# Local and pooled attention by half batches, with the local softmax on ScalarE and VectorE

## Chip, cores and metric

The kernel runs on one core of a Trainium2 chip (trn2). The metric is the device time of one execution in microseconds, lower is better.

## The reference

The input has 4 batches, 8 heads, 576 tokens and 64 features a head. The first layer adds a pooled and a local attention, and two feed-forward layers follow:

```python
q_d = q.reshape(B, H, Sd, 4, D).mean(axis=3)      # k_d, v_d likewise
out_up = np.repeat(softmax(scale * q_d @ k_d.T) @ v_d, 4, axis=2)
mask = np.abs(pos[:, None] - pos[None, :]) < 4
scores = np.where(mask, scale * q @ k.T, -1e9)
a = np.exp(scores - max(scores)); a = a / (sum(a) + 1e-09)
x = out_up + a @ v                                # -> 2304 tokens x 512
h = x @ w_in; g = s * relu(h)**2 + b; x = g @ w_out          # 512 -> 2048 -> 512
out = (x @ w_a) * (x @ w_b) @ w2                             # 512 -> 1536 -> 512
```

## The kernel before

Five engines run programs of their own, in the written order, and meet at semaphores. The work has three parts.

**Attention** works on pairs of heads: `n` from 0 to 15, four pairs to a batch. A pair has three jobs: POOLED (all 144 groups), LOCAL0 and LOCAL1 (three windows of 96 queries each, a half of the tokens; a window sees 102 keys). `turn` transposes q and k on TensorE, `take_turn` evacuates on ScalarE, `sum_groups` pools on VectorE. A job then goes through `scores` (TensorE), `maxima` (VectorE: add the mask, find the maximum), for a local job `subtract` (GpSimd), `exps` (ScalarE), `weigh` (VectorE: sum, add 1e-9, reciprocal), `normalise` (GpSimd), `p_turn` (TensorE), `take_p` (ScalarE), `values` (TensorE) and `take_values` (VectorE, into `xf`).

**The first feed-forward layer** runs in 128 slots: 8 chunks `c` of 288 tokens by 16 blocks `f` of 128 hidden features. Every float32 product is made of three matmuls of a high and a low part, so weights (`split_w_hi`, `split_w_lo`) and activations are split first. A slot has `up_matmuls` (12 matmuls into the one bank HB), `take_relu` and `split_g_hi` on ScalarE, `square` and `split_g_lo` on VectorE, and `down_matmuls` of the slot two before it. `up_matmuls` of a slot waits for `take_relu` of the one before.

**The last layer** has 72 steps (`up_2`, `down_2`); its weight blocks are loaded and split in the last slots (0 to 5), behind them (6 to 8) and beside the first steps (9 to 11).

Before slot 0 a boot of 30 ticks makes all of batch 0: pairs 0 to 3 in two sets of buffers, six ticks apart, and splits six of the 16 weight blocks. In slots 0 to 95 pairs 4 to 15 are made in one set of buffers, eight slots (16 half slots `at`) to a pair. In each engine's loop `attention(n, at)` for the even half comes ahead of `up_matmuls`, `take_relu` and `square`; the one for the odd half comes behind these and ahead of `down_matmuls`, `split_g_hi` and `split_g_lo`. The pair's banks are used again and again, so a step also waits until the bank is free: `scores` of LOCAL1 in half slot 9 waits for `take_values` of POOLED in half slot 8 (the tensor `up`). SyncE issues nearly all DMAs, in written order too.

In the last slots store and load of the layer's result pass through DRAM (`o_dram`).

Of the kernel before, what the change touches and what calls it, by code (L numbers as in the profile page):

```python
# [4 lines left out]
P = 128  # L5
# [15 lines left out]
GW = NW // 2  # L21
SC = D ** -0.5


POOLED, LOCAL0, LOCAL1 = 0, 1, 2
JOBS = 3
NP = PAIRS * B

BOOT_SKEW = 6
BOOT_END = 11
BOOT_TICKS = BOOT_SKEW * (PAIRS - 1) + BOOT_END + 1
BOOT_BLOCKS = 6
BOOT_BLOCK_TICKS = (10, 14, 18, 22, 25, 28)

NCH = 2 * B
SLOTS = NCH * F1
GB = 3
# [8 lines left out]
STAGES = 3  # L48


def build(nc, q, k, v, w_in, w_out, s, b, w_a, w_b, w2, mask_in, identity, out, o_dram):
# [6 lines left out]
    with stack:  # L58
# [5 lines left out]


        boot = ExitStack()
        nat1 = sb(boot, "nat1", [WQ, 2, NW, 2 * D])
        vnat1 = sb(boot, "vnat1", [GH, 2, POOL * 2 * D])
        vwin1 = sb(boot, "vwin1", [WK, NW, 2 * D])
        vd1 = sb(boot, "vd1", [GH, 2, 2 * D])  # L70
        qT1 = sb(boot, "qT1", [P, S])
        kT1 = sb(boot, "kT1", [P, S + 2 * HALO])
        pooledT1 = sb(boot, "pooledT1", [P, 2, G])
        sm1 = sb(boot, "sm1", [WQ, 3, 2 * GW * WK])
        pts1 = sb(boot, "pts1", [WK, 2, GW * WQ])
        up1 = sb(boot, "up1", [P, G])
        sm0b = sb(boot, "sm0b", [WQ, 2 * GW * WK])
# [5 lines left out]
        nat0 = sb(first, "nat0", [WQ, 2, NW, 2 * D])  # L83
        vnat0 = sb(first, "vnat0", [GH, 2, POOL * 2 * D])
        vwin0 = sb(first, "vwin0", [WK, NW, 2 * D])
        vd0 = sb(first, "vd0", [GH, 2, 2 * D])
        qT0 = sb(first, "qT0", [P, S])
        kT0 = sb(first, "kT0", [P, S + 2 * HALO])
        pooledT0 = sb(first, "pooledT0", [P, 2, G])
        sm0 = sb(first, "sm0", [WQ, 2, 2 * GW * WK])  # L90
        pts0 = sb(first, "pts0", [WK, 2, GW * WQ])
        up0 = sb(first, "up0", [P, G])
        mask = sb(first, "mask", [WQ, NW, WK])
        ident = sb(first, "ident", [P, P])
        stat = sb(first, "stat", [WQ, 2, JOBS, 3, 2 * GW])
        xf = sb(first, "xf", [P, PAIRS, S])
# [40 lines left out]

        def block2(part, f):
# [25 lines left out]
        kT_clear = sem("kT_clear")  # L164
        vwin_clear = sem("vwin_clear")
        nat_in = [sem("nat_in0"), sem("nat_in1")]
        vnat_in = [sem("vnat_in0"), sem("vnat_in1")]
        vwin_in = [sem("vwin_in0"), sem("vwin_in1")]
# [4 lines left out]
        turn_ready = sem("turn_ready")  # L173
        turn_taken = sem("turn_taken")
        pooled = sem("pooled")
        s_ready = sem("s_ready")
        masked = sem("masked")
        mx_ready = sem("mx_ready")
        shift_ready = sem("shift_ready")
        sub_ready = sem("sub_ready")  # L180
        exp_ready = sem("exp_ready")
        sum_ready = sem("sum_ready")
        eps_ready = sem("eps_ready")
        rec_ready = sem("rec_ready")
        p_ready = sem("p_ready")
        pt_ready = sem("pt_ready")
        pt_taken = sem("pt_taken")
        v_half = sem("v_half")
        vd_ready = sem("vd_ready")
        o_ready = sem("o_ready")  # L190
        o_taken = sem("o_taken")
# [31 lines left out]
        def alone(n):  # L223
            return n < PAIRS

        def kit(n):
            return n % 2 if alone(n) else 0

        def before(n):

            return n - 2 if n <= PAIRS else n - 1

        def uses(n):

            return n // 2 + 1 if alone(n) else n - PAIRS + 3

        def job(n, kind):

            return JOBS * n + kind + 1 if n >= 0 else 0

        def local(n, kind):
            return 2 * n + kind if n >= 0 else 0

        def nat(n):
            return (nat0, nat1)[kit(n)]

        def vnat(n):
            return (vnat0, vnat1)[kit(n)]

        def vwin(n):  # L250
            return (vwin0, vwin1)[kit(n)]

        def vd(n):
            return (vd0, vd1)[kit(n)]

        def qT(n):
            return (qT0, qT1)[kit(n)]

        def kT(n):
            return (kT0, kT1)[kit(n)]  # L260

        def pooledT(n):
            return (pooledT0, pooledT1)[kit(n)]

        def pts(n):
            return (pts0, pts1)[kit(n)]

        def up(n):
            return (up0, up1)[kit(n)]

        def sm_flat(n, kind):
            if kit(n):
                return sm1[:, kind]
            if kind < LOCAL1:
                return sm0[:, kind]
            return sm0b[:, :] if alone(n) else sm0[:, 0]

        def sm_pooled(n):
            return sm_flat(n, POOLED)[0:GH, 0:4 * G].rearrange("p (e f c) -> p e f c", e=2, f=2)

        def sm_local(n, kind):
            return sm_flat(n, kind).rearrange("p (e u c) -> p e u c", e=2, u=GW)

        def rows_of(kind):
            return GH if kind == POOLED else WQ

        def blocks_of(kind):
            return 4 if kind == POOLED else 2 * GW

        def mx(n, kind):  # L290
            return stat[0:rows_of(kind), kit(n), kind, 0, 0:blocks_of(kind)]

        def shift(n):
            return stat[0:GH, kit(n), POOLED, 1, 0:4]

        def den(n, kind):
            return stat[0:rows_of(kind), kit(n), kind, 2, 0:blocks_of(kind)]


        def turn_bank(n, t):  # L300
            return 4 * kit(n) + t if alone(n) else (0, 1, 2, 0)[t]

        def s_bank(n, kind):
            return 4 * kit(n) + (2 if kind == LOCAL0 else 0) if alone(n) else 0

        def pt_bank(n):
            return 4 * kit(n) + 2 if alone(n) else 1

        def o_bank(n, kind):
            return 4 * kit(n) + (1 if kind == LOCAL0 else 0) if alone(n) else 0  # L310

        def boot_tick(at, tick_of):

            return [p for p in range(PAIRS) if at - BOOT_SKEW * p == tick_of]

# [3 lines left out]
        def _(sp):  # L319
            def load_qk(n):  # L320
                i, p = divmod(n, PAIRS)
                past(sp, turn_ready, 4 * before(n) + 4)
                for t, a in enumerate((q, k)):
                    for e in range(2):
                        src = a[i, 2 * p + e].rearrange("(w t) d -> t w d", t=WQ)
                        sp.dma_start(nat(n)[:, t, :, e * D:(e + 1) * D], src).then_inc(nat_in[kit(n)], 16)

            def load_v(n):
                i, p = divmod(n, PAIRS)
                past(sp, vd_ready, before(n) + 1)  # L330
                groups = v.rearrange("b h (f g r) d -> b f g h (r d)", f=2, r=POOL)
# [825 lines left out]
```

## Time and profile before

| | us |
|---|---|
| median of 3 runs | 1069.96 (1068.77 to 1071.46) |
| profiled execution | 1069.81 |
| its span, first to last instruction | 1068.0 |
| busy: TensorE matmul | 1009.2 (94%) |
| busy: VectorE | 442.6 (41%) |
| busy: ScalarE | 356.3 (33%) |
| busy: GpSimd | 159.4 (15%) |

The span is what the trace shows, the execution's own time lies 1.8 us above it. The boot ends near 79 us, the last slot near 596 us, and the last layer takes the rest. A busy share is a mean over these parts. A line of the trace's timeline gives the start, the duration and the instruction; the brackets behind it hold how long the engine had been idle and whose event ended that. TensorE's granted clock is 1.00 at 2.4 GHz and 0.50 at 1.2 GHz.

### The profile page before, as it was taken

What the parts mean: (1) busy time and instruction counts of PE and PEld (TensorE: products, weight loads), DVE (VectorE), ACT (ScalarE), POOL (GpSimd) and SP (SyncE); (2) the same over time, 40 slices, a digit from 0 to 9 for tenths busy, and PEclk for the clock granted to TensorE, in tenths of its full rate; (3) what the DMA queues carried; (4) which work ended last, traced back from release to release, by engine and by line L of the source; (5) the groups of instructions that cost most, each with busy time, mean ns of one, the idle gap of its engine ahead of it and who ended that gap; (6) DMA issues with size and microseconds to landing.
All of it is one profiled execution on the core that took longest, in us unless ns stands there. A gap on an engine that the chain in (4) does not pass through costs nothing.

```text
span 1068.0 us, 17004 instructions
## 1 busy us (share of the span) xinstructions
PE 1009.2 (94%) x6984; PEld 944.7 (88%) x6984; DVE 442.6 (41%) x800; ACT 356.3 (33%) x791; POOL 159.4 (15%) x126
## 2 busy tenths in 40 slices
PE   5678899999999999999999799999999999999997
PEld 4557889999999999999999699899899898998996
DVE  4768665565555655554345521211211212112111
ACT  3445444444344443344245421211211212212211
POOL 4545343122331223310000000000000000000000
PEclk9659999999999999999999899999999999999999
DMA  7343401121011210201033600010100100100000
GB/s 193 77 124 112 126 20 50 45 68 46 17 52 46 68 46 15 55 13 43 10 111 119 200 1 1 20 40 1 57 3 1 60 1 1 60 1 1 30 2 30
DMA packets 98829, 52.50 MB, mean 49 GB/s; under 512 B 60384, under 2 KB 92768, under 8 KB 98752
## 3 DMA queue, kind: packets, MB, share of 16 engines
q1 hardware_dynamic: 98608, 51.35, 17.3%
q8 instruction: 55, 0.90, 0.4%
q14 instruction: 22, 0.18, 0.1%
q10 hardware_dynamic: 144, 0.07, 0.0%
HBM read 41.97 MB, written 9.44 MB: 48 GB/s over the span
## 4 chain that ended last, share of the span: by engine, by line
PE 85%; DVE 6%; ACT 3%; POOL 3%; issue 2%; DMA 1%; SPq 0%; ACTq 0%; DVEq 0%; POOLq 0%
PE bank L667 28%; PE bank L632 18%; PE bank L617 17%; PE bank L681 13%; PE bank L546 2%; PE bank L493 2%; PE bank L517 2%; PE bank L467 1%; DVE relu L992 1%; POOL sm L1073 1%; PE bank L478 1%; POOL sm L1081 1%; PE bank L538 1%; POOL wx L1088 1%; PE bank L512 1%
## 5 line engine op out<-in xcount | busy, mean ns | idle before, releaser
L667 PE MATMUL bank<-x_hi,wx 128*128 128x384 f32 x1152 | 307.0, 337 | 11.8 <-DVE prod L1051 7.8
L632 PE MATMUL bank<-g_hi,wx 128*128 128x288 f32 x1024 | 234.2, 305 | 1.4 <-DVE o_sb L1004 1.4
L617 PE MATMUL bank<-wx 128*128 128x288 f32 x1536 | 230.7, 299 | 0.4 <-ACT relu L792 0.4
L667 PEld LDWEIGHTS bank<-x_hi,wx 128*128 128x128 f32 x1152 | 210.2, 188 | 17.3 <-issue 14.4
L617 PEld LDWEIGHTS bank<-wx 128*128 128x128 f32 x1536 | 211.8, 190 | 3.4 <-issue 2.8
L667 PE MATMUL bank<-x_lo,wx 128*128 128x384 f32 x576 | 193.5, 336 | 0.0
L632 PEld LDWEIGHTS bank<-g_hi,wx 128*128 128x128 f32 x1024 | 171.9, 189 | 9.5 <-issue 4.2
L1051 DVE TENSOR_TENSOR prod<-bank,a_sb 128x384 f32<-128x384 f32 x72 | 40.1, 558 | 314.5 <-ACT a_sb L854 314.5
L632 PE MATMUL bank<-g_lo,wx 128*128 128x288 f32 x512 | 151.5, 296 | 0.0
L992 DVE SCALAR_TENSOR_TENSOR relu<-relu,s_col 128x288 f32<-128x288 f32 x128 | 81.7, 638 | 166.4 <-ACT relu L792 166.2
L854 ACT ACTIVATE a_sb<-bank 128x384 f32<-128x384 f32 x72 | 35.3, 491 | 303.7 <-PE bank L667 303.7
L681 PE MATMUL bank<-wx,p_hi 128*128 128x512 f32 x432 | 134.4, 392 | 0.0
L667 PEld LDWEIGHTS bank<-x_lo,wx 128*128 128x128 f32 x576 | 108.6, 188 | 2.8
L792 ACT ACTIVATE relu<-bank 128x288 f32<-128x288 f32 x128 | 52.6, 411 | 173.7 <-PE bank L617 173.7
L632 PEld LDWEIGHTS bank<-g_lo,wx 128*128 128x128 f32 x512 | 96.7, 189 | 0.0
L797 ACT ACTIVATE g_hi<-relu,b_col 128x288 fp32r<-128x288 f32 x128 | 68.5, 535 | 80.4 <-DVE relu L992 80.4
L1081 POOL TENSOR_TENSOR sm<-sm,stat 96x612 f32<-96x612 f32 (+1 forms) x46 | 56.3, 1224 | 246.5 <-DVE stat L900 246.5
L681 PEld LDWEIGHTS bank<-wx,p_hi 128*128 128x128 f32 x432 | 80.1, 188 | 13.4
L996 DVE SCALAR_TENSOR_TENSOR g_lo<-relu,b_col,g_hi 128x288 fp32r<-128x288 f32 x128 | 70.6, 552 | 41.7 <-ACT g_hi L797 41.7
L681 PE MATMUL bank<-wx,p_lo 128*128 128x512 f32 x216 | 85.5, 396 | 0.0
L1054 DVE TENSOR_TENSOR p_lo<-prod,p_hi 128x384 fp32r<-128x384 f32 x72 | 40.2, 559 | 42.6 <-ACT p_hi L857 42.6
L857 ACT ACTIVATE p_hi<-prod 128x384 fp32r<-128x384 f32 x72 | 37.8, 526 | 46.2 <-DVE prod L1051 46.2
(67 smaller groups left out, 821.4 us busy)
## 6 DMA issues: line engine op xcount, KB each, us to landing
nat<-in_q SPq DMA_DIRECT2D x32, 144.0 KB, 2.9
nat<-in_k SPq DMA_DIRECT2D x32, 144.0 KB, 3.2
vnat<-in_v SPq DMA_DIRECT2D x32, 144.0 KB
o_transposed<-o_sb SPq DMA_DIRECT2D x8, 576.0 KB, 3.2
o_raw<-o_transposed SPq DMA_DIRECT2D x6, 768.0 KB, 4.7
out<-y SPq DMA_DIRECT2D x18, 256.0 KB, 2.2
vwin<-in_v SPq DMA_DIRECT2D x32, 120.0 KB
raw<-in_moe_w_a SPq DMA_DIRECT2D x12, 256.0 KB, 3.1
```

The source lines that it names most:

```text
L617: mm = nc.tensor.matmul(HB[:, 0:HALF], wi(w, kd, f), xs(x, c % 2)[:, kd], start=(kd == 0 and j == 0), stop=(kd == KD - 1 and j == 2))
L632: mm = nc.tensor.matmul(ACC[o][:, 0:HALF], wo(w, f, o), g[:, slot % GB, :], start=(f == 0 and j == 0), stop=(f == F1 - 1 and j == 2))
L667: mm = nc.tensor.matmul(dst[:, 0:CH2], wab(w, f, j * KD + kd), x[:, kd, :], start=(kd == 0 and m == 0), stop=(kd == KD - 1 and m == 2))
L681: mm = nc.tensor.matmul(ACC[tt], x[:, f % GB, tt * P:(tt + 1) * P], rows2(w, f), start=(f == 0 and m == 0), stop=(f == F2 - 1 and m == 2))
L792: nc.scalar.activation(relu[:, slot % 2, :], HB[:, 0:HALF], ACT.Relu).then_inc(r_ready, 1)
L797: nc.scalar.activation(g_hi[:, slot % GB, :], relu[:, slot % 2, :], ACT.Identity, bias=b_col[:, 0:1])\
L857: nc.scalar.activation(p_hi[:, f % GB, :], prod[:, f % 2, :], ACT.Copy).then_inc(ph_ready, 1)
L992: nc.vector.scalar_tensor_tensor(r, r, s_col[:, 0:1], r, ALU.mult, ALU.mult).then_inc(q_ready, 1)
L996: nc.vector.scalar_tensor_tensor(g_lo[:, slot % GB, :], relu[:, slot % 2, :], b_col[:, 0:1], g_hi[:, slot % GB, :].bitcast(f32), ALU.add, ...
L1051: nc.vector.tensor_tensor(prod[:, f % 2, :], bank[:, 1, 0:CH2], a_sb[:, f % 2, :], ALU.mult)\
L1054: nc.vector.tensor_tensor(p_lo[:, f % GB, :], prod[:, f % 2, :], p_hi[:, f % GB, :].bitcast(f32), ALU.subtract).then_inc(pl_ready, 1)
L1081: nc.gpsimd.tensor_tensor(x, x, d, ALU.mult).then_inc(p_ready, 1)
```

## The change

The work of attention is cut anew. A unit `u` is a pair of heads over half a batch (288 tokens): its three local windows and its 72 pooled queries. There are 32; units 4c to 4c+3 feed chunk `c`. The first units of a pair (`leads`) also transpose all its keys and sum its pooled values, which are kept for the second half. The boot makes units 0 to 3 only, in four buffer sets (34 ticks), with four weight blocks; units 4 to 31 are made in the slots, eight half slots to a unit, each over some 15 ticks, so two units are in work at a time. Weight blocks 4 to 15 are split one to a slot in slots 0 to 11.

Scores are kept negated. The local maximum becomes a minimum and enters `exp` as a bias, so ScalarE makes six exponentials of 96x102 instead of one of 96x612 and `subtract` on GpSimd goes. The 1e-9 stands in a 103rd column that the sum takes in. The local `normalise` moves from GpSimd to VectorE, next to the reciprocal. `up` is taken by ScalarE (`take_up`) in place of VectorE. Loads of the windows are joined, the first loads are shared between two queues, and blocks 6 to 11 of the last layer are split behind the steps.

The core of the diff:

```diff
+NU = PAIRS * NCH
+SETS = PAIRS
+PER_UNIT = 2 * F1 // PAIRS
+LEAD = 3
 BOOT_SKEW = 6
+BOOT_TICKS = 34
+BOOT_BLOCK_TICKS = (-14, -9, -5, -3)
+EARLY2 = 6
...
+        def bank_before(u):
+            return max(u - 1, 0) if u <= PAIRS else u
+        def at_tick(g, boot_tick, tick):
+            first = [u for u in range(PAIRS) if BOOT_SKEW * u - BOOT_TICKS + boot_tick == g]
+            return first + [u for u in range(PAIRS, NU) if PER_UNIT * (u - PAIRS) - LEAD + tick == g]
...
         @block.tensor
+            def scores(u):
+                _, h, p = place(u)
+                at = base(u)
+                pe.wait_ge(kp_ready, pair(u) + 1)
+                pe.wait_ge(qp_ready, u + 1)
+                past(pe, ptl_taken, bank_before(u))
+                past(pe, o_taken, bank_before(u))
...
+            def attention(g):
+                for u in at_tick(g, 12, 7):
+                    values(u)
+                for u in at_tick(g, 0, -5):
+                    if leads(u):
+                        turn_k(u)
+                for u in at_tick(g, 1, -4):
+                    turn_q(u)
+                for u in at_tick(g, 3, 0):
+                    scores(u)
+                for u in at_tick(g, 11, 6):
+                    turn_pooled(u)
+                for u in at_tick(g, 10, 6):
+                    turn_local(u)
...
             for slot in range(SLOTS):
-                c, f = divmod(slot, F1)
-                n, at = PAIRS + slot // 8, 2 * (slot % 8)
-                attention(n, at)
-                if slot > 0:
-                    up_matmuls(c, f)
-                attention(n, at + 1)
+                attention(2 * slot)
+                up_matmuls(*divmod(slot, F1))
+                attention(2 * slot + 1)
                 if slot >= 2:
                     down_matmuls(*divmod(slot - 2, F1))
...
         @block.scalar
+            def exp_local(u):
+                act.wait_ge(mnl_ready, u + 1)
+                for j in range(2 * GW):
+                    x = kits[kit(u)]["sml"][:, j, 0:WK]
+                    done = nc.scalar.activation(x, x, ACT.Exp, bias=mnl(u)[:, j:j + 1], scale=-1.0)
+                done.then_inc(el_ready, 1)
...
+            def take_up(u):
+                act.wait_ge(o_ready, u + 1)
+                past(act, o_taken, before(u))
+                nc.scalar.activation(kits[kit(u)]["up"][:], bank[:, base(u) + 2, HALF:HALF + GH], ACT.Copy,
+                                     scale=1.0 / POOL).then_inc(up_taken, 1)
...
+            def attention(g):
+                for u in at_tick(g, 13, 8):
+                    take_up(u)
+                for u in at_tick(g, 14, 9):
+                    split_x_hi(u)
+                for u in at_tick(g, 12, 6):
+                    take_pooled(u)
+                for u in at_tick(g, 11, 6):
+                    take_local(u)
+                for u in at_tick(g, 1, -5):
+                    if leads(u):
+                        take_k(u)
+                for u in at_tick(g, 2, -4):
+                    take_q(u)
+                for u in at_tick(g, 6, 2):
+                    exp_local(u)
+                for u in at_tick(g, 8, 3):
+                    exp_pooled(u)
...
-            for f in range(6, 9):
-                split_w2_hi(f)
             take_acc(NCH - 1)
...
         @block.vector
+            def weigh_local(u):
+                dve.wait_ge(el_ready, u + 1)
+                nc.vector.tensor_reduce(denl(u), kits[kit(u)]["sml"][:], X, ALU.add).then_inc(sum_ready, 1)
+                dve.wait_ge(sum_ready, u + 1)
+                nc.vector.reciprocal(denl(u), denl(u)).then_inc(recl_ready, 1)
+                dve.wait_ge(recl_ready, u + 1)
+                x = kits[kit(u)]["sml"][:, :, 0:WK]
+                d = denl(u).unsqueeze(2).to_broadcast([WQ, 2 * GW, WK])
+                nc.vector.tensor_tensor(x, x, d, ALU.mult).then_inc(pl_done, 1)
+
+            def take_values(u):
+                dve.wait_ge(up_taken, u + 1)
+                past(dve, x_hi, u - 1)
+                past(dve, x_lo, u - 1)
+                dst = xf[:, u % 2, :].rearrange("p (g r) -> p g r", r=POOL)
+                src = bank[:, base(u) + 2, 0:HALF].rearrange("p (g r) -> p g r", r=POOL)
+                add = kits[kit(u)]["up"][:].unsqueeze(2).to_broadcast([P, GH, POOL])
+                nc.vector.tensor_tensor(dst, src, add, ALU.add).then_inc(o_taken, 1)
...
+            def attention(g):
+                for u in at_tick(g, 14, 8):
+                    take_values(u)
+                for u in at_tick(g, 15, 9):
+                    split_x_lo(u)
+                for u in at_tick(g, 1, -4):
+                    if leads(u):
+                        sum_k(u)
+                for u in at_tick(g, 2, -3):
+                    sum_q(u)
+                for u in at_tick(g, 4, 0):
+                    minima(u)
+                for u in at_tick(g, 8, 3):
+                    weigh_local(u)
+                for u in at_tick(g, 9, 4):
+                    weigh_pooled(u)
...
         @block.gpsimd
-            def subtract(n, kind):
...
-            def normalise(n, kind):
...
+            def attention(g):
+                for u in at_tick(g, 10, 5):
+                    normalise_pooled(u)
+                for u in at_tick(g, 5, -2):
+                    if leads(u):
+                        sum_v(u)
```

On SyncE `load_q`, `load_k`, `load_v` and `load_vwin` of unit u+1 are issued by the same ticks: queries, keys and values at tick -3 of unit u, windows at tick 8 of unit u. `store_o` of the last chunk is now issued ahead of the loads of blocks 9 to 11, not of 11 alone.

## Rows read from the trace of the kernel before

**Rows 1.** The page, part 1: busy us (share of the span) xinstructions.
```profile
PE 1009.2 (94%) x6984; PEld 944.7 (88%) x6984; DVE 442.6 (41%) x800; ACT 356.3 (33%) x791; POOL 159.4 (15%) x126
```

**Rows 2.** Timeline of TensorE, steady slots: start us, us, instruction.
```profile
255.93 0.91 PE L467 MATMUL bank<-ident,nat 96*128 96x96 f32 x9
289.24 0.91 PE L467 MATMUL bank<-ident,nat 96*128 96x96 f32 x9
...
492.89 1.75 PE L617 MATMUL bank<-wx 128*128 128x288 f32 x12
496.08 1.75 PE L617 MATMUL bank<-wx 128*128 128x288 f32 x12
```

**Rows 3.** Waits of TensorE, 78 to 200 us: total, times, longest.
```profile
PE bank L478 <- DVE pooledT L868: 3.3, 2, 1.9
PE bank L493 <- DVE up L907: 3.0, 2, 1.7
...
PE bank L617 <- ACT relu L792: 0.4, 1, 0.4
```

**Rows 4.** Timeline, boot: first transposes, first and last minimum search of a half.
```profile
6.82 2.15 PE L467 MATMUL bank<-ident,nat 96*128 96x96 f32 x12 [6.82 <-DMA nat<-in_k]
...
13.38 0.79 DVE L890 TENSOR_REDUCE stat<-sm 96x6 f32<-96x612 f32 x1
...
66.54 0.79 DVE L890 TENSOR_REDUCE stat<-sm 96x6 f32<-96x612 f32 x1
```

**Rows 5.** Forms by line, 200 to 600 us: xcount, busy us, mean ns.
```profile
L890 DVE TENSOR_REDUCE stat<-sm 96x6 f32<-96x612 f32 x18 | 14.2, 786 | 0.6
L888 DVE TENSOR_TENSOR sm<-bank,mask 96x612 f32<-96x612 f32 x18 | 14.0, 780 | 0.0
L719 ACT ACTIVATE sm<-sm 96x612 f32<-96x612 f32 x18 | 12.7, 704 | 0.0
L713 ACT ACTIVATE sm<-bank,stat 72x144 f32<-72x144 f32 x32 | 11.6, 370 | 3.4 <-DVE stat L877 3.4
L776 ACT ACTIVATE wx<-xf 128x288 fp32r<-128x288 f32 x24 | 10.4, 433 | 0.0
L868 DVE TENSOR_REDUCE pooledT<-kT 128x144 f32<-128x576 f32 x8 | 6.0, 748 | 0.0
```

**Rows 6.** Timeline of TensorE, first slots; in brackets the idle before.
```profile
85.11 1.85 PE L617 MATMUL bank<-wx 128*128 128x288 f32 x12
...
99.08 0.77 PE L493 MATMUL bank<-kT,qT 64*96 64x102 f32 x12 [1.75 <-DVE up L907]
```

**Rows 7.** Timeline around 254 us, TensorE, then ScalarE, then VectorE.
```profile
253.57 0.72 PE L546 MATMUL bank<-pts,vwin 102*64 102x96 f32 x12
...
253.68 0.41 ACT L792 ACTIVATE relu<-bank 128x288 f32<-128x288 f32 x1 [0.59 <-PE bank L617]
...
254.13 0.52 DVE L992 SCALAR_TENSOR_TENSOR relu<-relu,s_col 128x288 f32<-128x288 f32 x1 [1.02 <-ACT relu L792]
254.56 0.45 DVE L917 TENSOR_TENSOR xf<-bank,up 128x288 f32<-128x288 f32 x1
```

**Rows 8.** Timeline of VectorE: a 96x6 operation while GpSimd splits a block.
```profile
96.49 2.13 DVE L898 TENSOR_SCALAR stat<-stat 96x6 f32<-96x6 f32 x1
```

**Rows 9.** Windows of TensorE: length, busy (x), granted clock, DMA share, GB/s.
```profile
121.00:124.00 3.00, 1.09 (x11) 1.00 0.20 77
...
126.00:128.00 2.00, 2.00 (x10) 0.50 1.10 255
```

**Rows 10.** Timeline of TensorE, start of the last stage.
```profile
606.97 0.66 PE L667 MATMUL bank<-x_hi,wx 128*128 128x384 f32 x1 [6.56 <-DVE prod L1051]
...
613.95 0.41 PE L667 MATMUL bank<-x_hi,wx 128*128 128x384 f32 x1 [1.26 <-DVE prod L1051]
```

**Rows 11.** The chain that ended last, same place: start us, us, what.
```profile
606.97 5.73 PE bank L667 x24
...
620.43 4.18 PE bank L667 x24
```

More of the change, by code:

```diff
@@ L306, in pt_bank, with place, leads, pair @@
[L306 to L314, printed above, removed]
+        def place(u):
+            return u // (2 * PAIRS), u // PAIRS % 2, u % PAIRS
+        def leads(u):
+            return place(u)[1] == 0
+        def pair(u):
+            i, _, p = place(u)
+            return PAIRS * i + p
@@ L319, in _, with load_q @@
         def _(sp):
[L320 to L330, printed above, removed]
+            def load_q(u, heads=range(2)):
+                i, h, p = place(u)
+                past(sp, q_turned, before(u))
+                for e in heads:
+                    src = q[i, 2 * p + e, h * HALF:(h + 1) * HALF].rearrange("(w t) d -> t w d", t=WQ)
+                    sp.dma_start(kits[kit(u)]["natq"][:, :, e * D:(e + 1) * D], src).then_inc(q_in[kit(u)], 16)
@@ L457, in _ @@
         def _(pe):
-            def turn(n, t):
-                if t == 0:
-                    pe.wait_ge(nat_in[kit(n)], 64 * uses(n))
-                    past(pe, o_taken, job(before(n), LOCAL1))
-                    past(pe, pt_taken, job(before(n), LOCAL1))
-                if t == 3 and not alone(n):
-                    pe.wait_ge(turn_taken, 4 * n + 1)
-                for u in range(GW):
-                    mm = nc.tensor.transpose(bank[:, turn_bank(n, t), u * WQ:(u + 1) * WQ],
-                                             nat(n)[:, t // 2, GW * (t % 2) + u, :], ident[0:WQ, 0:WQ])
-                mm.then_inc(turn_ready, 1)
@@ new lines, in turn_local @@
+            def turn_local(u):
+                pe.wait_ge(pl_done, u + 1)
+                if not alone(u) and u + 1 < NU:
+                    pe.wait_ge(q_taken, u + 2)
+                for e in range(2):
+                    for w in range(GW):
+                        mm = nc.tensor.transpose(bank[0:WK, base(u) + e, w * WQ:(w + 1) * WQ],
+                                                 kits[kit(u)]["sml"][:, GW * e + w, 0:WK], ident[0:WQ, 0:WQ])
+                mm.then_inc(ptl_ready, 1)
@@ new lines, in take_q, with exp_pooled @@
+            def take_q(u):
+                act.wait_ge(q_turned, u + 1)
+                past(act, sl_ready, before(u))
+                nc.scalar.activation(kits[kit(u)]["qT"][:], bank[:, turn_q_bank(u), 0:HALF], ACT.Copy, scale=-SC)\
+                  .then_inc(q_taken, 1)
+            def exp_pooled(u):
+                act.wait_ge(shift_ready, u + 1)
+                past(act, ptp_ready, before(u))
+                for e in range(2):
+                    done = nc.scalar.activation(kits[kit(u)]["smp"][:, e], bank[0:GH, base(u) + 2, e * G:(e + 1) * G],
+                                                ACT.Exp, bias=shift(u)[:, e:e + 1], scale=-1.0 / POOL ** 2,
+                                                accum_out=denp(u)[:, e:e + 1])
+                done.then_inc(ep_ready, 1)
@@ L1036, in _ @@
                         split_w2_lo(f // 2 - 2)
-            for f in range(6, 9):
-                split_w2_lo(f)
             take_acc(NCH - 1)
@@ L1124 @@
+            for g in range(-BOOT_TICKS, 0):
+                attention(g)
+                if g in BOOT_BLOCK_TICKS and BOOT_BLOCK_TICKS.index(g) % 2 == 1:
+                    split_w_lo(BOOT_BLOCK_TICKS.index(g))
+            for slot in range(SLOTS):
+                c, f = divmod(slot, F1)
+                attention(2 * slot)
+                attention(2 * slot + 1)
+                if c == 0 and f + BOOT_BLOCKS < F1 and f % 2 == 1:
+                    split_w_lo(f + BOOT_BLOCKS)
 _INS = ['q', 'k', 'v', 'moe_w_in', 'moe_w_out', 'moe_s', 'moe_b', 'moe2_w_a', 'moe2_w_b', 'moe2_w_out']
```

886 lines of the change are left out of this document (328 added, 558 removed).

## The prediction

> **What bounds the kernel now.** I read the engine shares first, then the waits of TensorE, then whole slots. TensorE is busy for 94% of the span [rows 1], so in the main loops the time is TensorE's own work plus the gaps in it. A slot without attention takes 496.08 - 492.89 = 3.19 us. Eight slots with one pair's attention take 289.24 - 255.93 = 33.31 us [rows 2], so a pair costs 33.31 - 8 x 3.19 = 7.79 us of TensorE, and there is no gap in that stretch. The pair is spread over 11 interludes between products; its matmuls alone add up to about 6.2 us in the same stretch, which leaves about 0.14 us for each change between attention and products (an estimate from these rows).
>
> The other losses lie in three places. First, the boot, where VectorE, ScalarE and GpSimd pass small tiles to each other: the first search for a local maximum ends at 14.2 us, the last but none of the eight starts at 66.54 [rows 4], and the third up product, the first from which the loop is full, starts at 85.11 [rows 6]. Second, the first twenty slots: seven kinds of waits, 11.8 us between 78 and 200 us [rows 3], of which 10.0 lie behind 85.11, and about 1.7 us for matmuls at half clock behind the longest gap [rows 9]. Third, the entry of the last stage: a gap of 6.56 us and then matmuls that begin at 0.66 us apiece instead of 0.41 [rows 10].
>
> **The boot shrinks: -24 us.** The change does only the first half of batch 0 before slot 0: four units in four buffer sets, each half a pair. Per unit VectorE has the mask (0.78), the minimum (0.79), a reduction of the keys (0.75) [rows 5], a sum of the minimum's size, and smaller ones: I take 6.3 us with the new multiply, which bounds a unit from below. The chain is longer than that, because the engines work in written order. From one unit's local minimum to the next one's: six exponentials 1.5, take_up 0.2, take_k 0.6, sum_k 0.7, take_values 0.4, x_hi 0.4, take_q 0.3, sum_q 0.4, weigh_local 1.9, x_lo 0.4, weigh_pooled 0.4, mask and minimum 1.6, and thirteen handovers of some 0.07: 9.7 us. The first minimum ends earlier than now, since only the first keys must be there before the first transpose (now all four loads are, at 6.8 us [rows 4]): I take 11.1. Three units on, with 2 us for the weight splits in between, is 42. From the last unit's minimum to the third up product come its exponentials, weights, transposes, values, take_values and split (14 us, unit 4's scores and minima are queued ahead of take_values on VectorE), then two up products that no down product covers (5 us): 61 us, against 85.11 now, so -24.1. A chain of 7.5 us a unit gives 53, one of 12 gives 68: the term lies in -32 to -17.
>
> **More attention in the loop: +13.5 us.** Now 12 pairs run in the slots; after, 28 half units (14 pairs). The matmuls of a unit are half a pair's, except that the pooled values take four products of 72 columns instead of two of 144 (0.05 us more); interludes fall from 11 to 9 for two units. Two units: 6.33 + 9 x 0.14 = 7.6, a unit 3.8 (3.6 to 4.1). Behind the third up product: 28 x 3.8 less 1.4 for unit 4's queries and scores in the boot = 105; now 12 x 7.79 less 2.0 = 91.5. Bounds +8 to +22.
>
> **The exchanges of engines: nothing on the path.** The two GpSimd operations on each half's local block (subtract, normalise) go. The subtraction becomes the bias of six exponentials over 102 columns in place of one over 612 (0.704 us [rows 5]). No row has 96x102; the pooled ones of 72x144 take 0.37 us, and 288 against 612 elements (0.43, 0.70) give 0.8 ns an element [rows 5], so I take 0.3 us each, with starts 0.25 apart: 1.5 us in all. Bounds 1.2 and 2.2 (six times 0.37). The multiply on VectorE is a 96x612 operation like the mask: 0.79. ScalarE then works about 9 and VectorE about 11 us in a unit's 16.6 us, so neither is the bound. From the scores (tick 0) to the transposes (tick 6) lie three slots, about 12 us, for mask to multiply of some 7 us plus their places in the queues; placing them against relu, square and g_hi, I find the pooled probabilities ready 1.7 us before TensorE asks. If the exponentials took 2.2 this cover falls to 1.0 and still holds. The local epsilon in a 103rd column saves a small operation off the path.
>
> The page "ScalarE: Activation LUTs" of the Trainium skill (Rules for kernel authors) budgets about 0.3 us per ACTIVATE plus 0.83 ns per element. By that six would cost 2.3 us, which speaks against this part; the boot would be some 3 us longer and the sum 1093.
>
> **The handover between units: +40 us.** This term decides. Unit u+1's scores sit at tick 0, an odd half slot, behind the up product of that slot, and wait for o_taken of unit u, because their banks are the same. o_taken comes from take_values at tick 8, the same half slot. values of unit u are done before that up product, but take_up is queued on ScalarE behind take_relu of the slot, and take_values on VectorE behind square, and both of these wait for the up product. So TensorE finishes it and then waits for relu, square, take_values. The same three stand in a row now: TensorE starts its next group at 253.57, relu starts 253.68, square 254.13, take_values 254.56 and ends 255.01 [rows 7]. Now nobody waits for them. With 0.05 us to TensorE that is 255.06 - 253.57 = 1.49 us; take_up (0.2 us, from 253.98) hides beside square. Units 5 to 31 pay it: 27 x 1.49 = 40.2 us. The row nearest to it is the wait of LOCAL1's scores for up in the first slots, 1.75 us [rows 6], where VectorE was also held back by GpSimd. Queued behind the waiting scores is the down product of the slot, which has been ready for long, so it can't fill the gap. Bounds 1.35 and 2.0 us: +36 to +54.
>
> **The first slots: -2.7 us.** The weight splits keep their place (one in each of slots 0 to 11, now ten in slots 2 to 11). A 96x6 operation of VectorE took 2.13 us while GpSimd was splitting [rows 8]. GpSimd's other work is mostly gone, but each unit's chain is longer, and normalise_pooled stands behind a split. I take 9 us for 11.7 (4 to 16: -8 to +4).
>
> **The last stage: -6.9 us.** Blocks 6 to 8 are no longer split ahead of the first a_sb; they follow step by step beside 6 us of products. The 6.56 us gap becomes 1.26, as at the next step [rows 10], and the half clock goes with it (5.73 against 4.18 us for 24 matmuls [rows 11]): 5.3 + 1.55. Loads move on SP too: store_o now waits ahead of three block loads rather than one, and these are due many steps later. Bounds -7 to -5.
>
> **Sum.** -24.1 + 13.5 + 40.2 - 2.7 - 6.9 = +20.0 us. The profiled execution took 1069.8 us (span 1068.0, 1.8 around it), the median of three is 1069.96. Forecast 1069.8 + 20 = 1090 us.
>
> **Rivals.** (1) *No gap at the handover.* take_values is done before TensorE asks, or the gap only moves one that would be there anyway: 1090 - 40 = 1050, faster. For it: in 200 to 300 us every such dependence of the present order is met in time. Against it: now the evacuation sits in an even half slot, ahead of square in VectorE's queue; in the change it is behind it, in program order, which engines don't pass by. 12%.
> (2) *The gaps drop the clock.* Behind a gap of 1.91 us the granted clock stood at 0.50 in 126 to 128 us, that is 1.2 GHz [rows 9]; 1.7 us were lost. At each of 27 handovers that is +46: 1136. Against it: four other gaps of 1.3 to 1.8 us, the one in rows 6 among them, were followed by matmuls at 2.4 GHz. Decides if a 1.5 us gap is enough. 4%.
> The page "TensorE: Matmul & The Clock Gate" (the HAM clock gate) holds that the half rate is the idle default and activity lifts it; gaps this short beside dense work would then seldom do it.
> (3) *A shorter boot than thought.* If VectorE's own work bounds it (6.3 us a unit) the loop is full at 50, the sum 1079: inside the main case.
>
> **Chances.** The main case 82%, its own range 1067 to 1115 from the bounds above, which don't all fall on one side. Rival 1: 12%, rival 2: 4%, another way 2%. The range 1068 to 1115 leaves out both rivals and little of the main case. This kernel's runs tell a change from none at about 0.3%, 3.2 us: faster 0.14, same 0.04, slower 0.82.
>
> **What would show it.** The waits of TensorE list the scores line waiting for xf from take_values, 27 times, about 1.5 us, evenly until some 540 us. Four slots with one unit take 18 us, not 16.6. The third up product starts near 61. The entry to the last stage has no gap over 1.5 us. POOL's busy time falls to well under half. I am wrong in the main point if the scores start right behind the up product.

## The result, and the profile after

The changed kernel takes 1088.68 us (median of four runs, 1086.81 to 1088.80) against 1070.71 us before on the same chip (four runs, 1068.77 to 1073.02). The ratio is 1.0163, interval 1.0143 to 1.0184: slower by 1.6%. The profiled execution took 1088.69 us, its span 1086.9. The forecast was 1090.

The page of the changed kernel, parts 1 and 5 (busy us, share, instructions; then a group with its busy time, mean ns, and the idle time before it with what ended it):

```profile
PE 1001.5 (92%) x7112; PEld 941.4 (87%) x7112; DVE 447.1 (41%) x866; ACT 387.5 (36%) x983; POOL 76.4 (7%) x80
...
L498 PE MATMUL bank<-pooledk,pooledq 64*72 64x144 f32 x128 | 30.0, 318 | 48.1 <-DVE xf L862 42.7
```

Against [rows 1], GpSimd's busy time has halved (159.4 to 76.4), ScalarE works 31 us more, and TensorE is busy for 7.7 us less in a span 18.9 us longer: the time is in gaps. Where the gaps are is in the waits of TensorE in the changed kernel (total, times, longest):

```profile
PE bank L498 <- DVE xf L862: 42.7, 27, 2.1
PE bank L484 <- ACT kT L658: 5.8, 5, 2.9
PE bank L523 <- POOL smp L983: 5.5, 5, 1.5
...
PE bank L533 <- DVE sml L853: 3.7, 1, 3.7
...
PE bank L627 <- DVE prod L958: 2.5, 2, 1.3
```

L498 is the first matmul of a unit's scores, L862 is take_values. It waits 27 times, once for each of units 5 to 31. The timeline of the changed kernel at one of these handovers (start, us, instruction, idle before):

```profile
310.31 1.86 PE L585 MATMUL bank<-wx 128*128 128x288 f32 x12
312.21 0.41 ACT L744 ACTIVATE relu<-bank 128x288 f32<-128x288 f32 x1 [3.21 <-PE bank L585]
312.52 0.22 ACT L697 ACTIVATE up<-bank 128x72 f32<-128x72 f32 x1
312.66 0.52 DVE L907 SCALAR_TENSOR_TENSOR relu<-relu,s_col 128x288 f32<-128x288 f32 x1 [3.10 <-ACT relu L744]
313.09 0.45 DVE L862 TENSOR_TENSOR xf<-bank,up 128x288 f32<-128x288 f32 x1
313.69 0.31 PE L498 MATMUL bank<-pooledk,pooledq 64*72 64x144 f32 x1 [1.51 <-DVE xf L862]
```

The up product ends, relu starts, square starts, take_values starts behind it, and only then may the scores begin. It is the row of [rows 7] with somebody waiting at its end. Both engines in between are otherwise idle (3.21 and 3.10 us before their instructions).

The boot and the entry of the last stage answer to [rows 4], [rows 6], [rows 10] and [rows 11]. The timeline of the changed kernel, first and last minimum search of the boot, and the third up product:

```profile
11.28 0.79 DVE L831 TENSOR_REDUCE stat<-sml 96x6 f32<-96x612 f32 x1
...
40.84 0.79 DVE L831 TENSOR_REDUCE stat<-sml 96x6 f32<-96x612 f32 x1
...
66.44 1.86 PE L585 MATMUL bank<-wx 128*128 128x288 f32 x12
```

The chain that ended last in the changed kernel, at the entry of the last stage (start, us, what):

```profile
616.90 5.00 PE bank L597 x36
621.90 4.21 PE bank L627 x24
627.36 4.42 PE bank L627 x24
```

The third up product starts at 66.44 instead of 85.11 [rows 6], and the last stage has no gap like the 6.56 us of [rows 10]: the 24 matmuls of its second step, which stood behind that gap, take 4.42 us, where [rows 11] had 5.73.

### The profile page after: what moved, and what is told of

Same layout as the page of the kernel before. It is cut to its first block, busy times and chain, and to the rows that moved or that the text cites. A ratio compares the mean times of both kernels' runs of the same rounds, so it can differ in the third digit from the quotient of the medians.

```text
span 1086.9 us, 17677 instructions
## 1 busy us (share of the span) xinstructions
PE 1001.5 (92%) x7112; PEld 941.4 (87%) x7112; DVE 447.1 (41%) x866; ACT 387.5 (36%) x983; POOL 76.4 (7%) x80
## 4 chain that ended last, share of the span: by engine, by line
PE 88%; DVE 5%; ACT 4%; issue 2%; POOL 1%; DMA 1%; DVEq 0%; ACTq 0%; POOLq 0%
PE bank L627 28%; PE bank L597 19%; PE bank L585 18%; PE bank L641 13%; PE bank L550 2%; PE bank L498 2%; PE bank L533 2%; PE bank L504 1%; DVE xf L862 1%; PE bank L543 1%; ACT relu L744 1%; PE bank L523 1%; DVE sml L853 1%; PE bank L471 1%; ACT sml L679 1%
## 5 line engine op out<-in xcount | busy, mean ns | idle before, releaser
L907 DVE SCALAR_TENSOR_TENSOR relu<-relu,s_col 128x288 f32<-128x288 f32 x128 | 73.1, 571 | 123.9 <-ACT relu L744 123.9
L498 PE MATMUL bank<-pooledk,pooledq 64*72 64x144 f32 x128 | 30.0, 318 | 48.1 <-DVE xf L862 42.7
L498 PEld LDWEIGHTS bank<-pooledk,pooledq 64*72 64x72 f32 x128 | 15.3, 153 | 55.0 <-issue 55.0
L961 DVE TENSOR_TENSOR p_lo<-prod,p_hi 128x384 fp32r<-128x384 f32 x72 | 40.2, 558 | 42.5 <-ACT p_hi L801 42.5
```

Of the source, the lines that this page charges most:

```text
L498: return nc.tensor.matmul(bank[0:GH, at + 2, e * G:(e + 1) * G], kits[kit(u)]["pooledq"][rows, :], pooledk[rows, p, :], start=True, stop=True)
L907: nc.vector.scalar_tensor_tensor(r, r, s_col[:, 0:1], r, ALU.mult, ALU.mult).then_inc(q_ready, 1)
L961: nc.vector.tensor_tensor(p_lo[:, f % GB, :], prod[:, f % 2, :], p_hi[:, f % GB, :].bitcast(f32), ALU.subtract).then_inc(pl_ready, 1)
```

## The experiments

In each, `...` stands for lines that stay. A ratio is against the kernel before on the same chip; for differences among the variants I use their medians. They ran on different chips, on which the kernel before had medians of 1068.4 to 1070.7 us, so a difference under some 2 us can't be told.

**1. Both evacuations half a slot earlier (take_early).** The theory: take_values stands behind square in VectorE's queue, so it comes late for a bank that TensorE asks for at once. If both steps move one tick ahead, nothing stands behind them and the gap goes.

```diff
-                for u in at_tick(g, 13, 8):
+                for u in at_tick(g, 13, 7):
                     take_up(u)
...
-                for u in at_tick(g, 14, 8):
+                for u in at_tick(g, 14, 7):
                     take_values(u)
```

> The changed kernel with one edit: take_up and take_values of a unit at tick 7 instead of 8, that is in the even half slot, ahead of take_relu and square in their engines' queues. Theory (handover): o_taken comes while the up product still runs, the 27 waits of the scores for take_values (42.7 us in the profile of the changed kernel) go, nothing takes their place: 1089 - 43 = 1046 us, below the kernel before. Rival (the gaps only hide others, TensorE is then late at the next wait, for the pooled probabilities or for relu): the waits reappear under another name and the time falls by under 15 us, to 1074 or more.

Measured 1041.02 us, ratio 0.9735 (0.9720 to 0.9749): 47.7 us below the changed kernel and 2.7% below the kernel before. The timeline of this run at a handover:

```profile
301.73 1.86 PE L585 MATMUL bank<-wx 128*128 128x288 f32 x12
301.85 0.23 ACT L697 ACTIVATE up<-bank 128x72 f32<-128x72 f32 x1 [1.44 <-PE bank L550]
302.11 0.46 DVE L862 TENSOR_TENSOR xf<-bank,up 128x288 f32<-128x288 f32 x1 [1.15 <-ACT up L697]
303.52 0.34 PE L498 MATMUL bank<-pooledk,pooledq 64*72 64x144 f32 x1
```

take_values now runs beside the up product and is done 0.95 us before the scores start. The wait of L498 for L862 isn't in the list of this run, and between 200 and 560 us the only wait of TensorE left is one of 0.3 us. So nothing was queued behind the gap to take its place. The gaps were 42.7 us, and half clock behind two of them in the first slots (below) is about 3 us more. The other 2 us are in the handovers too. From the scores at 151.59 to those at 546.23 us the changed kernel takes 394.6 us, with 22 handovers; this run takes 359.8 for the same stretch (138.96 to 498.80). That is 1.58 us for each, 0.07 more than the gap in the trace, because here the scores begin 0.07 us before the up product ends.

**2. Which of the two must move.** take_up alone, then take_values alone.

```diff
-                for u in at_tick(g, 13, 8):
+                for u in at_tick(g, 13, 7):
                     take_up(u)
```

> The changed kernel with take_up alone moved to tick 7 (ahead of take_relu on ScalarE), take_values left at tick 8 behind square. Theory: relu, square and take_values are what TensorE waits for, take_up only lay beside square; the 27 gaps stay at 1.5 us: 1089 us, within 2. Rival (take_up is part of the chain): it falls by 27 x 0.2 = 6 us.

Measured 1087.86 us, ratio 1.0174 (1.0156 to 1.0193); the wait is 42.9 us, as in the changed kernel. The copy on ScalarE was hidden beside square, as the prediction said.

```diff
-                for u in at_tick(g, 14, 8):
+                for u in at_tick(g, 14, 7):
                     take_values(u)
```

> The changed kernel with take_values alone at tick 7 (ahead of square on VectorE), take_up left behind take_relu on ScalarE. Theory: the chain becomes relu, take_up, take_values, by the starts in the changed kernel's rows 0.31 + 0.2 + 0.45 and handovers, 1.2 us in place of 1.5: 1089 - 8 = 1081 us, and it needs take_up's move too to get rid of the rest (41 us more, as take_early showed with both). Rival (VectorE's place alone decides): near 1041.

Measured 1077.32 us, ratio 1.0078 (1.0058 to 1.0097), the wait 32.5 us. Moved alone, take_values still needs the copy, which stands behind relu; its place in front of square is worth only 0.3 us a handover. The timeline of take_values_only:

```profile
303.73 0.23 ACT L697 ACTIVATE up<-bank 128x72 f32<-128x72 f32 x1
303.99 0.46 DVE L862 TENSOR_TENSOR xf<-bank,up 128x288 f32<-128x288 f32 x1 [3.22 <-ACT up L697]
304.37 0.51 DVE L907 SCALAR_TENSOR_TENSOR relu<-relu,s_col 128x288 f32<-128x288 f32 x1
304.60 0.31 PE L498 MATMUL bank<-pooledk,pooledq 64*72 64x144 f32 x1 [1.20 <-DVE xf L862]
```

The gap goes only when both queues let their step pass. Each edit alone gives 0.8 and 11.4 us, the two together 47.7.

**3. The gap made longer (gap_longer, gap_small).** Rival 2 said that the gaps drop the clock. In the changed kernel they don't in the steady slots. Is the 1.51 us gap near to where they would? A reduction on VectorE that nobody reads, just ahead of take_values, makes it longer: over 96x408 elements (0.57 us), then over 96x102 (0.25 us).

```diff
                 for u in at_tick(g, 14, 8):
+                    if not alone(u):
+                        nc.vector.tensor_reduce(spare[:], mask[:], X, ALU.add)
                     take_values(u)
```

> The changed kernel with one more operation on VectorE ahead of each take_values of units 4 to 31: a sum over the mask (96 x 408) into a spare tile that nobody reads, about 0.55 us. It changes nothing that is computed. Theory: each of the 27 handover gaps grows by 0.5 us to some 2.05 us: 1089 + 14 = 1103 us. Rival (clock): gaps of 2.1 us, as the three in the first slots of the changed kernel, of which two were followed by a granted clock near half, bring 1.2 GHz behind many of them, at 1.7 us each: up to 1103 + 46 = 1149 us, and windows with a granted clock well below 1.00 all over the slots.

Measured 1129.74 us, ratio 1.0562 (1.0546 to 1.0578): 41.1 us more than the changed kernel, where the waits grew by 12.3 (42.7 to 55.0). Windows of TensorE (length, busy, granted clock, DMA share, GB/s), of gap_longer and then of the changed kernel:

```profile
312.00:316.00 4.00, 3.92 (x27) 0.57 0.13 44
160.00:260.00 100.00, 90.02 (x754) 0.93 0.11 28
260.00:360.00 100.00, 90.03 (x756) 0.93 0.18 46
```

```profile
200.00:300.00 100.00, 90.92 (x825) 1.00 0.18 48
300.00:400.00 100.00, 92.44 (x835) 1.00 0.14 36
```

At 312 us stands a handover of gap_longer with a gap of 2.00 us; in the next 4 us the clock was granted at 0.57, that is 1.2 GHz for most of them. Whether a handover is followed by such a stretch can be read from the time to the next scores. Two units in a row in gap_longer, the first without and the second with half clock before it ends:

```profile
272.90:291.70 18.80, 16.81 (x151) 1.00 0.19 48
291.70:312.00 20.30, 18.37 (x151) 0.92 0.25 67
```

From 136 us on, 17 of the 23 intervals from scores to scores are 1.5 us longer in this way. That makes 26 of the 41.1 - 12.3 = 28.8 us that aren't waits.

> As gap_longer, with a sum over 96 x 102 instead of 96 x 408 ahead of take_values, about 0.2 us, so gaps of 1.7 us instead of 1.5 and 2.0. gap_longer cost 41 us for gaps 13.5 us longer in sum, the rest being matmuls at half clock. Theory A (the clock falls only behind gaps near 2 us): 1089 + 27 x 0.2 = 1094 us, granted clock 1.00 in steady slots. Theory B (any lengthening brings some of it, in proportion): 1089 + 15 = 1104 us, granted clock 0.97 or so.

For gap_small the same reduction runs over `mask[:, 0:1, :]`. Measured 1103.61 us, ratio 1.0320 (1.0302 to 1.0339), 14.9 us more than the changed kernel; the waits grew by 4.2, so about 10.7 us are clock. Of the same 23 intervals 7 are 1.5 us longer, which makes 10.7; in the changed kernel none is. One handover of gap_small, then its windows:

```profile
302.32 0.31 PE L499 MATMUL bank<-pooledk,pooledq 64*72 64x144 f32 x1 [1.68 <-DVE xf L863]
```

```profile
160.00:260.00 100.00, 91.62 (x828) 1.00 0.14 36
260.00:360.00 100.00, 89.95 (x784) 0.97 0.16 42
```

In the steady slots the clock stood at 1.00 throughout with gaps of 1.51 us, at 0.97 to 1.00 with 1.68 us and at 0.93 to 0.95 with 2.00 us. To price a gap of 1.5 us at its own length was right, with less than 0.2 us to spare.

**4. The multiply on GpSimd (mult_gpsimd).** What did the multiply by the reciprocal on VectorE, the change's own step, bring? In this run the units and their order stay, and only the multiply goes back to GpSimd.

```diff
-                nc.vector.tensor_tensor(x, x, d, ALU.mult).then_inc(pl_done, 1)
...
+            def normalise_local(u):
+                pool.wait_ge(recl_ready, u + 1)
+                x = kits[kit(u)]["sml"][:, :, 0:WK]
+                d = denl(u).unsqueeze(2).to_broadcast([WQ, 2 * GW, WK])
+                nc.gpsimd.tensor_tensor(x, x, d, ALU.mult).then_inc(pl_done, 1)
...
             def attention(g):
+                for u in at_tick(g, 8, 3):
+                    normalise_local(u)
                 for u in at_tick(g, 10, 5):
                     normalise_pooled(u)
```

> The changed kernel with the multiply of the local probabilities back on GpSimd, right behind the reciprocal (tick 3), the rest as it is. Theory (this part lies off the path in the slots): no new wait in steady slots; in the boot the multiply takes 1.2 instead of 0.8 us and holds small operations of VectorE: 1089 + 2 to + 5, so 1091 to 1094 us. Rival (the move to VectorE is what costs or brings the time): over 10 us either way.

Measured 1099.54 us (1096.38 to 1101.87), ratio 1.0285 (1.0257 to 1.0312): 10.9 us worse, above what was expected. The waits of TensorE in mult_gpsimd:

```profile
PE bank L498 <- DVE xf L858: 40.9, 27, 1.5
PE bank L523 <- POOL smp L979: 12.7, 17, 3.0
...
PE bank L533 <- POOL sml L985: 5.5, 4, 4.4
```

The pooled normalise stands behind the multiply on GpSimd, so TensorE waits 17 times for the pooled probabilities, 12.7 us instead of 5.5. The same edit on top of take_early (early_mult_gpsimd) shows it without the handover's gap:

> take_early with the local multiply back on GpSimd (both edits together). In the changed kernel this edit cost 11 us, 7 of them as new waits of TensorE for the pooled probabilities, whose operations on VectorE and GpSimd stand behind the multiply or behind a square held by it. Theory: TensorE now comes to these waits no later, so they cost at least as much: 1041 + 9 to + 15, 1053 us. Rival (the cost came with the handover gap, where everything is late): 1041 to 1045 us.

Measured 1058.83 us (1053.54 to 1059.44), ratio 0.9892 (0.9864 to 0.9921): 17.8 us worse than take_early, above the 9 to 15 us expected. Windows of early_mult_gpsimd, then of take_early:

```profile
60.00:80.00 20.00, 17.95 (x116) 0.66 0.33 95
80.00:100.00 20.00, 16.99 (x141) 0.91 0.40 117
100.00:120.00 20.00, 16.97 (x141) 0.91 0.43 125
```

```profile
60.00:80.00 20.00, 18.74 (x145) 0.86 0.33 96
80.00:100.00 20.00, 17.68 (x160) 1.00 0.49 146
100.00:120.00 20.00, 18.44 (x172) 1.00 0.38 95
```

The waits grow by 7.1 (L523) + 1.8 (L533) + 0.5 (relu) = 9.4 us, the lower clock costs 20 x (0.20 + 0.09 + 0.09) = 7.6: together 17.0 of the 17.8. I had priced the waits and not what follows them. So the multiply's place is a gain of the change, 11 to 18 us in these two kernels, and it is the handover that turns the change's sum into a loss: with it the kernel is 18 us slower than before, without it (take_early) 29 us faster.

**5. The splits of the last layer at their old place (late_split).**

```diff
+            for f in range(6, 9):
+                split_w2_hi(f)
...
-                    if c == 0 and EARLY2 + f < F2:
-                        split_w2_hi(EARLY2 + f)
...
+                    if c == 0 and 9 + f < F2:
+                        split_w2_hi(9 + f)
```

The same on VectorE for the low parts, and the loads in their old order.

> The changed kernel with weight blocks 6 to 8 of the last layer split ahead of its first step again, and 9 to 11 ahead of steps 0 to 2, as in the kernel before. Theory: the gap of some 6.6 us at the second step comes back with a stretch at half clock: 1089 + 6.9 = 1096 us. Rival (the gap came from the loads, not from the splits' place): within 2 us of 1089.

Measured 1094.22 us, ratio 1.0232 (1.0215 to 1.0248): 5.5 us more than the changed kernel (4.2 between the two profiled executions), below the 6.9 expected. The waits of late_split have the old gap again, 5.6 us where the changed kernel has 1.3:

```profile
PE bank L626 <- DVE prod L963: 6.8, 2, 5.6
```

In the chain of late_split this gap ends behind the load of a weight block and the two halves of its split:

```profile
621.94 4.04 DMA raw<-in_moe_w_out
```

The run puts back the splits' place and the order of the loads together, so it doesn't say what each of them costs. The rival of its expectation, the loads, is not ruled out by it.

**6. The boot and the exponentials, on take_early.** Four runs ask where the loop could start earlier.

In early_boot the second boot block is split three ticks later:

```diff
-BOOT_BLOCK_TICKS = (-14, -9, -5, -3)
+BOOT_BLOCK_TICKS = (-14, -6, -5, -3)
```

> take_early with the second weight block of the boot split at tick -6 instead of -9 (GpSimd then splits behind the last unit's pooled normalise and not beside its local multiply). In the changed kernel that multiply took 2.59 us instead of 0.79 beside the split, and TensorE waited 3.7 us for it. Theory (GpSimd's split holds the multiply, on the boot's chain): the multiply takes 0.8 us, the slots begin 1.5 to 2.5 us earlier: 1039 us. Rival (the boot has slack there): 1041, no change.

The reason is this stretch of the changed kernel's timeline, where the fourth unit's multiply meets GpSimd's split of that block:

```profile
45.10 2.36 POOL L996 TENSOR_TENSOR wx<-stage,wx 128x1024 fp32r<-128x1024 f32 x1 [2.22 <-ACT wx L729]
45.52 2.59 DVE L853 TENSOR_TENSOR sml<-sml,stat 96x612 f32<-96x612 f32 x1
48.17 1.20 PE L533 MATMUL bank<-ident,sml 96*102 96x96 f32 x6 [3.69 <-DVE sml L853]
```

Measured 1040.32 us (1038.96 to 1041.61), ratio 0.9721 (0.9696 to 0.9746): no difference from take_early can be told. The mechanism is there, but the gain isn't: the multiply takes 0.79 us, TensorE waits 1.9 instead of 3.7 and the first up product starts 1.3 us earlier (53.37 for 54.70), yet the third up product ran at half rate (3.03 us from 65.76) and the next began at 71.37, where take_early's began at 71.03.

In early_one_exp one exponential over 96x612 takes the place of the six:

```diff
-                for j in range(2 * GW):
-                    x = kits[kit(u)]["sml"][:, j, 0:WK]
-                    done = nc.scalar.activation(x, x, ACT.Exp, bias=mnl(u)[:, j:j + 1], scale=-1.0)
+                x = kits[kit(u)]["sml"][:, :, 0:WK]
+                done = nc.scalar.activation(x, x, ACT.Exp, scale=-1.0)
```

> take_early with one exponential of 96 x 612 in place of six of 96 x 102; it leaves out the subtraction of the maximum (the minimum is still searched), so this piece of the computation is missing. Theory (the six are hidden in the slots, and stand on the chain of the boot only, once a unit): 1.7 us become 0.7, four to five times: 1041 - 3 to - 5, 1037 us. Rival (they cost ScalarE time that the slots feel): over 10 us less, as 32 units give 32 us.

Measured 1036.43 us, ratio 0.9687 (0.9660 to 0.9714): 4.6 us below take_early, half of it before the third up product (64.21 for 66.58). One row of the changed kernel's timeline gives the price of six, against 0.70 for one in [rows 5]:

```profile
300.12 1.72 ACT L679 ACTIVATE sml<-sml,stat 96x102 f32<-96x102 f32 x6
```

In early_pooled_first VectorE weighs the pooled scores ahead of the sums and minima of its list:

```diff
+                for u in at_tick(g, 9, 4):
+                    weigh_pooled(u)
                 for u in at_tick(g, 1, -4):
...
                 for u in at_tick(g, 8, 3):
                     weigh_local(u)
-                for u in at_tick(g, 9, 4):
-                    weigh_pooled(u)
```

> take_early with weigh_pooled ahead of sum_k, sum_q, minima and weigh_local in VectorE's order of a half slot. The pooled probabilities come 0.4 to 0.7 us earlier behind units whose half slot has sum_k. Theory: TensorE's waits for them in the first slots (4.0 us, three times) shrink by 1 to 2 us and steady slots stay: 1039 to 1041 us, same within what can be told. Rival (the order of the four matters elsewhere, as for the exponentials of the next unit in the boot): slower by 2 us or more.

Measured 1038.08 us (1037.97 to 1040.51), ratio 0.9705 (0.9681 to 0.9730); the waits for the pooled probabilities fall from 5.5 to 4.7 us. At the edge of what can be told.

Both edits together, early_all:

> take_early with both the later split of the boot and weigh_pooled first: the two gains add, if each is real: 1041 - 2 - 1 = 1038 us. If either is none, 1039 to 1041.

Measured 1036.19 us (1036.07 to 1036.69), ratio 0.9683 (0.9661 to 0.9706). It is the fastest kernel here that computes the whole reference: 3.2% below the kernel before, 4.8 us below take_early. Here the third up product starts at 64.27 and runs at full rate (1.86 us). Why the same boot edit lowers the clock in one kernel and not in the other stays open.

## Why the prediction was right, point by point

The forecast was +20.0 us; the profiled executions differ by 1088.69 - 1069.8 = 18.9. The main term is right for the reason given. That the sum comes so near is partly luck: the boot and the handover cost 5.4 and 2.5 us more than forecast, the attention in the loop and the first slots about 7 and 1 us less.

- **The handover: forecast +40.2, measured 42.7.** The steady gap is 1.51 us (forecast 1.49): 20 of them between 200 and 560 us make 30.3. The mechanism and its count of 27 are as forecast. Of the other 2.5 us some 2 lie in the first slots, where three gaps were 2.1 us: square took 1.1 us instead of 0.52 there while GpSimd was splitting a block. Run 1 shows the term by itself.
- **Rival 1 (no gap)** was wrong for the reason given, the order of the queues. Run 1 shows that one tick would have made it right: its 1050 us were the forecast less this term, and the run gave 1041.
- **Rival 2 (the clock)** was rightly not the main case, but 4% was too little. At 1.51 us the clock held, in the steady slots. But behind two of the 2.1 us gaps of the first slots it stood at 0.63 (72 to 76 us) and 0.57 (92 to 96), and the runs of part 3 show how near the steady gap was. By four harmless gaps of up to 1.8 us the forecast argued that short gaps are safe; with 27 gaps of 1.68 us that would have been wrong by 10 us. The page "TensorE: Matmul & The Clock Gate" of the Trainium skill describes this too ("A second HAM failure mode: psum-queue depth-cycling"): short idles between groups of matmuls can send the gate back and forth. By that paragraph the rival deserved more; gap_longer agrees with it, the steady slots of the changed kernel don't.
- **The boot: forecast -24.1, measured 66.44 - 85.11 = -18.7.** Up to the last minimum the chain was right: forecast to end at 42, it ended at 41.63, after a first one at 12.07 (forecast 11.1). What failed is the tail behind it, 19 us in the forecast and 24.8 in the trace. The multiply cost 2.59 us instead of 0.79 while GpSimd split a block, TensorE waited 3.7 us, and the transposes and the second up product ran at half clock (1.20 us for six instead of 0.66; 3.25 for twelve instead of 1.85). In early_boot, where the multiply took 0.79 us again, the third up product began only 0.8 us earlier than in take_early, so the slow multiply alone doesn't explain the 5.8 us; how the rest divides isn't shown. The term lies within its bounds of -32 to -17, near their end.
- **More attention in the loop: forecast +13.5, measured +6 to +8.** This is the term that was mis-sized. A unit's price is as forecast: from one unit's scores to the next's is 17.62 or 18.33 us in turn; less the gap and four slots of 3.19 [rows 2] that is 3.35 and 4.06, 3.7 on average (forecast 3.8). The count was wrong. The forecast put 28 units behind the third up product, less 1.4 us for unit 4's queries and scores. But all of unit 4 stands ahead of that product, its transposes and its values too. In the changed kernel's timeline:

```profile
63.59 0.68 PE L523 MATMUL bank<-ident,smp 72*72 72x72 f32 x4
...
65.79 0.72 PE L550 MATMUL bank<-ptl,vwin 102*64 102x96 f32 x12 [0.34 <-ACT ptl L691]
```

  So 27 units remain, less some 0.3 us (an estimate) for unit 5's query transposes: 27 x 3.7 - 0.3 = 99.6 instead of 105. Less the 91.5 of before that is +8.1; what the whole stretch leaves for it (next point) is +6.5.
- **The first slots: forecast -2.7, measured about -3.6.** "I take 9 us for 11.7" was near. The waits other than the handover's between 66 and 200 us are 4.7 (L523 4.0, L484 0.4, L550 0.3), and half clock costs 4 x (0.06 + 0.37 + 0.43) = 3.4 between 68 and 76 and from 92 to 96 us: 8.1 us. As a check, the stretch between the third up product and the last stage is 510.95 us before (85.11 to 596.06) and 555.46 after (66.44 to 621.90): +44.5. Less 42.7 for the handover, with 3.6 for this point and 1.1 for shorter waits for o_sb (1.4 before, 0.3 after) added back, +6.5 is left for the attention. The 1.6 us between 6.5 and 8.1 I can't place.
- **The last stage: forecast -6.9, measured -7.0.** It takes 465.0 us for 472.0. Run 5 gives 4.2 to 5.5 us of it for the place of the splits and the order of the loads together.
- **The exchanges of engines: forecast 0 on the path.** In the steady slots right, with two sizes off. The six exponentials take 1.72 us, not 1.5, with starts 0.27 apart, so the estimate of 2.3 us by the page "ScalarE: Activation LUTs" of the Trainium skill (Rules for kernel authors), which adds up six whole instructions, was further off than mine. And the pooled probabilities were not ready 1.7 us early: GpSimd ends them at 306.87, and the load of their first transpose, L523 just below, had already waited 0.21 us for them. In the trace weigh_pooled stands on VectorE behind a square (0.51 us) and the keys' sum (0.74 us) and starts at 305.58 only.

```profile
306.01 0.86 POOL L983 TENSOR_TENSOR smp<-smp,stat 72x288 f32<-72x288 f32 x1 [15.31 <-DVE stat L842]
...
306.93 0.28 PEld L523 LDWEIGHTS bank<-ident,smp 72*72 72x72 f32 x4 [0.21 <-POOL smp L983]
```

So the cover that the prediction named was already used up. Run 4 shows its price when it is overdrawn.

## What to carry to other kernels

When work on a bank is to start right behind a large product, the step that frees the bank must stand in its engine's queue ahead of everything that waits for that product; look at each queue that the freeing passes through, since one that blocks keeps most of the gap. Read it off the timeline of the kernel before, where the same three instructions stand in a row with nobody waiting, and multiply by the count: a gap of 1.5 us was 4% of this kernel, and one tick of order gave it back. And test the margin to the half clock by making a gap a little longer, before a neighbouring edit does it for you.

## What was not expected of the hardware

- **Short gaps in dense work and the clock.** With 1.51 us of idle time every 17.6 to 18.3 us no gap of the steady slots was followed by half clock; with 1.68 us 7 of 23 were, with 2.00 us 17 of 23, at 1.5 us each. The half microsecond that gap_longer adds to a gap cost three times itself. In the first slots one gap of 2.05 us (113 us) was followed by a clock of 1.00, and in [rows 9] one of 1.91 us by half clock. Why one gap of a length is followed by 1.2 GHz and another isn't, these runs don't show.
- **VectorE beside GpSimd.** Some operations of VectorE that start while GpSimd works on a large block end only after it: the 96x612 multiply took 2.59 us instead of 0.79 beside a split of 2.36, square 1.37 instead of 0.52 beside GpSimd's multiply of 1.21. [rows 8] is a third case. Others aren't held: in the changed kernel four minimum searches (0.79 us) and four reciprocals (0.19 us) that began beside work of GpSimd took their usual time. The second case in mult_gpsimd's timeline:

```profile
309.04 1.21 POOL L985 TENSOR_TENSOR sml<-sml,stat 96x612 f32<-96x612 f32 x1 [13.11 <-DVE stat L849]
309.19 1.37 DVE L903 SCALAR_TENSOR_TENSOR relu<-relu,s_col 128x288 f32<-128x288 f32 x1 [0.23 <-ACT relu L744]
```

The page "SBUF — State Buffer" of the Trainium skill ("Who interferes with whom") says that only the pair of ports that the two engines share causes contention, and calls it an exclusive lock. The held operations agree with it.
